# Rotary attention and MLP on one core: query-key scores as three pairs of 64-row products in place of four 128-row ones

## The reference, cut to what matters

```python
q_rot, k_rot = (rotate(q), rotate(k))
scores = scale * np.matmul(q_rot, k_rot.transpose(0, 1, 3, 2))
scores = scores - np.max(scores, axis=-1, keepdims=True)
attn = np.exp(scores)
attn = attn / (np.sum(attn, axis=-1, keepdims=True) + 1e-09)
x = attn @ v                       # heads side by side: 2304 x 512
h = x @ w_in                       # 512 x 2048
g = h * np.tanh(softplus(h))
out = g @ w_out                    # 2048 x 512
```

## Time and profile before

| what | value |
|---|---|
| median of 3 runs | 749.82 us (747.87 to 752.75) |
| profiled execution, its own time | 751.79 us |
| its span, first to last instruction | 750.0 us |
| mean granted TensorE clock | 0.993 of full |
| PE busy | 713.9 us, 95% |
| PE weight loads busy | 668.4 us, 89% |
| DVE busy | 482.9 us, 64% |
| ACT busy | 554.2 us, 74% |
| POOL busy | 350.0 us, 47% |
| scores, matmuls of line 577 | 640, busy 121.0 us in all |

### The profile page before, as it was taken

How to read it: one execution, slowest core, us unless ns; L and a number is a source line. 1 busy time by engine, 2 the same in 40 slices (tenths; PEclk the granted TensorE clock), 3 DMA queues, 4 the chain that set the end, 5 groups by cost and what they waited for, 6 DMA issues and landing times.

```text
span 750.0 us, 16092 instructions
## 1 busy us (share of the span) xinstructions
PE 713.9 (95%) x5098; PEld 668.4 (89%) x5098; DVE 482.9 (64%) x697; ACT 554.2 (74%) x999; POOL 350.0 (47%) x341
## 2 busy tenths in 40 slices
PE   1899999999999999889799999999999999999998
PEld 1799999999999999879699988999988999988996
DVE  4699999999999999977663433443443443533341
ACT  1799999999999999767777666656657567476653
POOL 4988888888888888761420303112031120301000
PEclk9999999999999999999899999999999999999999
DMA  3136633333333333365210202002020210200000
GB/s 86 41 75 189 189 81 80 79 78 79 77 74 80 80 81 80 82 193 192 84 29 29 85 29 57 28 30 81 28 84 0 84 28 28 84 28 0 0 28 28
DMA packets 89956, 52.30 MB, mean 70 GB/s; under 512 B 65456, under 2 KB 79408, under 8 KB 89936
## 3 DMA queue, kind: packets, MB, share of 16 engines
q1 hardware_dynamic: 89936, 52.03, 25.8%
HBM read 37.78 MB, written 14.23 MB: 69 GB/s over the span
## 4 chain that ended last, share of the span: by engine, by line
PE 85%; DVE 7%; issue 3%; ACT 3%; POOL 1%; DMA 0%; SPq 0%; DVEq 0%; POOLq 0%; ACTq 0%
PE ps_pv L614 11%; PE ps_s L577 9%; PE ps_t L595 9%; PE ps_y L698 9%; PE ps_y L699 9%; PE ps_y L700 9%; PE ps_h L680 8%; PE ps_h L679 8%; PE ps_h L678 8%; PE ps_t L563 4%; DVE neg_max L894 1%; DVE v_st L910 1%; DVE xt L920 1%; DVE gl L1003 1%; ACT prob L749 1%
## 5 line engine op out<-in xcount | busy, mean ns | idle before, releaser
L993 DVE TENSOR_TENSOR h_sb<-h_sb,m_sb 128x1024 f32<-128x1024 f32 x36 | 58.0, 1611 | 200.7 <-ACT m_sb L820 200.7
L680 PE MATMUL ps_h<-xb_h,win_lo 128*128 128x256 f32 x576 | 163.0, 283 | 0.0
L679 PE MATMUL ps_h<-xb_l,win_hi 128*128 128x256 f32 x576 | 163.0, 283 | 0.0
L678 PE MATMUL ps_h<-xb_h,win_hi 128*128 128x256 f32 x576 | 163.0, 283 | 0.0
L761 ACT ACTIVATE ph<-ps_t 128x320 fp32r<-128x320 f32 (+3 forms) x256 | 117.4, 470 | 12.5 <-PE ps_t L595 10.7
L595 PE MATMUL ps_t<-id_f,prob 128*128 128x128 f32 x800 | 125.3, 275 | 0.6 <-DVE rt_early L936 0.2
L894 DVE TENSOR_REDUCE neg_max<-ps_s 128x1 f32<-128x576 f32 (+1 forms) x160 | 119.1, 744 | 6.2 <-PE ps_s L577 6.2
L577 PE MATMUL ps_s<-qkt 128*128 128x288 f32 x640 | 121.0, 312 | 1.9 <-ACT prob L749 1.3
L749 ACT ACTIVATE prob<-ps_s,neg_max 128x576 f32<-128x576 f32 (+1 forms) x160 | 118.3, 739 | 3.8 <-DVE neg_max L894 2.9
L698 PE MATMUL ps_y<-wout_hi,gh 128*128 128x512 f32 x288 | 113.4, 394 | 4.2 <-DVE gl L1003 4.2
L614 PE MATMUL ps_pv<-ph,v_st 128*128 128x256 f32 (+1 forms) x320 | 106.8, 345 | 9.6 <-DVE xt L920 9.1
(11 more groups left out here) (63 smaller groups left out, 1306.7 us busy)
## 6 DMA issues: line engine op xcount, KB each, us to landing
x_transposed<-xt SPq DMA_DIRECT2D x64, 144.0 KB, 2.4
x_raw<-x_transposed SPq DMA_DIRECT2D x9, 512.0 KB, 4.0
x_more<-x_transposed SPq DMA_DIRECT2D x9, 512.0 KB, 4.9
x_more<-reciprocals SPq DMA_DIRECT2D x18, 256.0 KB, 3.7
v_raw<-v_in SPq DMA_DIRECT2D x32, 128.0 KB, 2.2
win_raw<-w_in SPq DMA_DIRECT2D x4, 1024.0 KB, 6.0
wout_raw<-w_out SPq DMA_DIRECT2D x4, 1024.0 KB, 9.1
y_out<-y_sb SPq DMA_DIRECT2D x8, 512.0 KB, 2.8
```

Of the source, the lines that this page charges most:

```text
L678: nc.tensor.matmul(o, wh, xb_h[:, c, :], start=(c == 0), stop=False)
L679: nc.tensor.matmul(o, wh, xb_l[:, c, :], start=False, stop=False)
L680: mm = nc.tensor.matmul(o, wl, xb_h[:, c, :], start=False, stop=(c == KC - 1))
```

## The change

The lo·lo product is left out. The three others are each made as a pair of products of 64 rows: the one on the upper 64 rows takes the first 288 keys, the one on the lower 64 rows the other 288. They write different PSUM banks. For this the queries lie as [hi; lo] and [lo; hi], the keys as [first half; second half], once high and once low. That gives six matmuls of 64 rows and 288 columns a query tile, each with its weight load, for four of 128 rows.

What else moves: `qk_st` becomes `q_st` and `k_st`; `Q` on POOL becomes five instructions in place of three (two copies, two subtractions, one copy, each of 320 values a partition, where two were of 640); `K3` has 6 transposes in place of 3; the copies out of PSUM write other places, with as many values; the columns that `T` reads are permuted; the first head's split on DVE has 5 instructions for 3, and one more small memset.

```diff
-        qk_st = sb1("qk_st", [P, 2, NT, 3, D], F32R)
+        q_st = sb1("q_st", [P, NT, 3, D], F32R)
+        k_st = sb1("k_st", [P, 2 * NT + 1, D], F32R)
...
-                nc.gpsimd.tensor_scalar(qk_st[:, :, :, 0, :], rot[:, e], 1.0, 1.0, ALU.mult,
-                                        ALU.mult).then_inc(qk_hi, 1)
-                pool.wait_ge(qk_hi, h)
-                nc.gpsimd.tensor_tensor(qk_st[:, :, :, 1, :], rot[:, e], qk_st[:, :, :, 0, :].bitcast(F32),
+                nc.gpsimd.tensor_scalar(q_st[:, :, 0, :], rot[:, e, 0], 1.0, 1.0, ALU.mult, ALU.mult).then_inc(qk_hi, 1)
+                nc.gpsimd.tensor_scalar(k_st[:, 0:NT, :], rot[:, e, 1], 1.0, 1.0, ALU.mult, ALU.mult).then_inc(qk_hi, 1)
+                pool.wait_ge(qk_hi, 2 * h - 1)
+                nc.gpsimd.tensor_tensor(q_st[:, :, 1, :], rot[:, e, 0], q_st[:, :, 0, :].bitcast(F32),
                                         ALU.subtract).then_inc(qk_parts, 1)
-                nc.gpsimd.tensor_scalar(qk_st[:, 0, :, 2, :], qk_st[:, 0, :, 0, :].bitcast(F32), 1.0, 1.0,
+                pool.wait_ge(qk_hi, 2 * h)
+                nc.gpsimd.tensor_tensor(k_st[:, NT:2 * NT, :], rot[:, e, 1], k_st[:, 0:NT, :].bitcast(F32),
+                                        ALU.subtract).then_inc(qk_parts, 1)
+                nc.gpsimd.tensor_scalar(q_st[:, :, 2, :], q_st[:, :, 0, :].bitcast(F32), 1.0, 1.0,
                                         ALU.mult, ALU.mult).then_inc(qk_parts, 1)
...
+                elif j == 2:
+                    for n, first in enumerate((0, 2, NT, NT + 2)):
+                        src = k_st[:, first:first + 2, :].rearrange("p t d -> p (t d)")
+                        mm = nc.tensor.transpose(bank[:, n * P:n * P + P], src, id_r[:])
+                else:
+                    for n, (low, part) in enumerate((low, part) for low in range(2) for part in range(3)):
+                        if part < 2:
+                            first = low * NT + 3 + part
+                            src = k_st[:, first:first + 2, :].rearrange("p t d -> p (t d)")
+                        else:
+                            src = q_st[:, 4, low:low + 2, :].rearrange("p a d -> p (a d)")
+                        mm = nc.tensor.transpose(bank[:, n * TAIL:n * TAIL + P], src, id_r[:])
...
-                for stack in range(2):
-                    for part in range(2):
-                        mm = nc.tensor.matmul(ps_s[:, buf, part, 0:S // 2], qkt[:, e, stack, t * P:t * P + P],
-                                              qkt[:, e, 2, part * (S // 2):(part + 1) * (S // 2)],
-                                              start=(stack == 0), stop=(stack == 1))
+                for n, (q_low, k_low) in enumerate(((0, 0), (0, 1), (1, 0))):
+                    for side in range(2):
+                        rows = slice(side * D, side * D + D)
+                        stack = q_low if side == 0 else 1 - q_low
+                        first = (D, HALF)[side]
+                        mm = nc.tensor.matmul(ps_s[:, buf, side, 0:S // 2],
+                                              qkt[rows, e, stack, Q_COL[t]:Q_COL[t] + P],
+                                              qkt[rows, e, k_low, first:first + S // 2],
+                                              start=(n == 0), stop=(n == 2))
...
-            nc.vector.tensor_copy(qk_st[:, :, :, 0, :], turned).then_inc(first_steps, 1)
+            nc.vector.tensor_copy(q_st[:, :, 0, :], turned[:, 0]).then_inc(first_steps, 1)
+            nc.vector.tensor_copy(k_st[:, 0:NT, :], turned[:, 1]).then_inc(first_steps, 1)
```

More of the change, by code:

```diff
@@ L54 @@
 NTB = 3
+K_FIRST = (0, 2 * P + TAIL, P, 3 * P + TAIL, 2 * P)
+QK_BLOCK = 320
+Q_COL = (384, 512, 704, 832, 640)
 def order(text):
@@ L231, in attention_mlp @@
         rot = sb1("rot", [P, 2, 2, NT, D])
-        qk_st = sb1("qk_st", [P, 2, NT, 3, D], F32R)
+        q_st = sb1("q_st", [P, NT, 3, D], F32R)
+        k_st = sb1("k_st", [P, 2 * NT + 1, D], F32R)
         v_raw = sb1("v_raw", [P, NT, D])
         v_st = sb1("v_st", [P, 2, NT, 2, D], F32R)
-        qkt = sb1("qkt", [P, 2, 3, NT * P], F32R)
+        qkt = sb1("qkt", [P, 2, 2, 3 * QK_BLOCK], F32R)
         id_f = sb1("id_f", [P, P])
@@ L444, in rotate @@
                 if due(h - 2):
-                    pool.wait_ge(qk_parts, 2 * (h - 2))
+                    pool.wait_ge(qk_parts, 3 * (h - 2))
                 nc.gpsimd.tensor_tensor(rot[:, e], part_c[:], part_s[:], ALU.add).then_inc(rope_done, 1)
@@ L556, in qk_turn @@
                     if due(h):
-                        pe.wait_ge(qk_parts, 2 * h)
+                        pe.wait_ge(qk_parts, 3 * h)
                     else:
[L559 to L563, removed]
+                        pe.wait_ge(first_steps, 9)
+                if j < 2:
+                    for t in range(4):
+                        src = q_st[:, t, j:j + 2, :].rearrange("p a d -> p (a d)")
+                        mm = nc.tensor.transpose(bank[:, t * P:t * P + P], src, id_r[:])
+                elif j == 2:
[10 more added lines that the diff above has]
+                        mm = nc.tensor.transpose(bank[:, n * TAIL:n * TAIL + P], src, id_r[:])
                 mm.then_inc(kt_done, 1)
@@ L592, in p_turn @@
                         col = j * nq + (qt - CHUNK_TILES[chunk][0]) * P
-                        first = min(kt * P, S - P)
+                        first = K_FIRST[kt] if kt < 4 else K_FIRST[4] - TAIL
                         src = prob[:, e, qt, first:first + P]
@@ L651, in _ @@
             pe.wait_ge(pads_cleared, 1)
-            pe.wait_ge(prob_pads, 1)
+            pe.wait_ge(prob_pads, 2)
             start, pairs, end = parts(PE_STEP)
@@ L733, in take_qk @@
                         act.wait_ge(s_done, NT * (h - 1))
+                blocks = qkt[:, e, :, :].rearrange("p a (b x) -> p a b x", x=QK_BLOCK)
                 src = ps_t[:, bank, :]
-                if j < 3:
-                    dst = qkt[:, e, j, 0:FULL]
-                else:
-                    src, dst = src[:, 0:3 * P].rearrange("p (a q) -> p a q", a=3), qkt[:, e, :, FULL:FULL + P]
+                if j == 0:
+                    src, dst = src.rearrange("p (b x) -> p b x", b=2), blocks[:, 0, 1:3, D:QK_BLOCK]
+                elif j == 2:
+                    src, dst = src.rearrange("p (a x) -> p a x", a=2), blocks[:, :, 0, D:QK_BLOCK]
+                else:
+                    src = src[:, 0:6 * TAIL].rearrange("p (a b x) -> p a b x", a=2, b=3)
+                    dst = blocks[:, :, :, 0:TAIL]
                 nc.scalar.activation(dst, src, ACT.Copy).then_inc(kt_taken_a, 1)
@@ L872, in _ @@
             dve.wait_ge(first_steps, 4)
-            nc.vector.tensor_copy(qk_st[:, :, :, 0, :], turned).then_inc(first_steps, 1)
-            dve.wait_ge(first_steps, 5)
-            nc.vector.tensor_tensor(qk_st[:, :, :, 1, :], turned, qk_st[:, :, :, 0, :].bitcast(F32),
+            nc.vector.tensor_copy(q_st[:, :, 0, :], turned[:, 0]).then_inc(first_steps, 1)
+            nc.vector.tensor_copy(k_st[:, 0:NT, :], turned[:, 1]).then_inc(first_steps, 1)
+            dve.wait_ge(first_steps, 6)
+            nc.vector.tensor_tensor(q_st[:, :, 1, :], turned[:, 0], q_st[:, :, 0, :].bitcast(F32),
                                     ALU.subtract).then_inc(first_steps, 1)
-            nc.vector.tensor_copy(qk_st[:, 0, :, 2, :], qk_st[:, 0, :, 0, :].bitcast(F32)).then_inc(first_steps, 1)
-            dve.wait_ge(first_steps, 7)
+            nc.vector.tensor_tensor(k_st[:, NT:2 * NT, :], turned[:, 1], k_st[:, 0:NT, :].bitcast(F32),
+                                    ALU.subtract).then_inc(first_steps, 1)
+            nc.vector.tensor_copy(q_st[:, :, 2, :], q_st[:, :, 0, :].bitcast(F32)).then_inc(first_steps, 1)
+            dve.wait_ge(first_steps, 9)
             nc.vector.memset(prob[TAIL:P, 1, 4, :], 0.0).then_inc(prob_pads, 1)
+            nc.vector.memset(k_st[:, 2 * NT, :].bitcast(F32), 0.0).then_inc(prob_pads, 1)
             dve.wait_ge(id_loaded, 16)
@@ L888, in take_q @@
                     dve.wait_ge(s_done, NT * (h - 1))
-                nc.vector.tensor_copy(qkt[:, e, 1, 0:FULL], ps_t[:, SLOT_OF["K", 1] % NTB, :]).then_inc(kt_taken_v, 1)
+                dst = qkt[:, e, 1, :].rearrange("p (b x) -> p b x", x=QK_BLOCK)[:, 1:3, D:QK_BLOCK]
+                nc.vector.tensor_copy(dst, ps_t[:, SLOT_OF["K", 1] % NTB, :].rearrange("p (b x) -> p b x", b=2)
+                                      ).then_inc(kt_taken_v, 1)
             def row_max(h, e, t):
```

## The result

The changed kernel takes 785.12 us (median of 4, 784.72 to 787.13) against 751.29 us before on the same chip: 1.0465 times as long, interval 1.0423 to 1.0508. The profiled execution has a span of 785.1 us against 750.0. The forecast was 744.0 with a range to 766: wrong in sign and outside the range.

The account below looks back on a forecast made before the run. PE, DVE and ACT were taken as near their limit together, POOL's loop bounding the new steps at 9.2 us. 751.8 - 7.5 (steps) + 0.5 (early steps) + 1.0 (start) = 745.8; against the median, 2 less, 744.0; range 738 to 766.

Parts of the forecast that it names:

- Three engines near the limit, so a saving is bounded: Attention stage: PE, DVE and ACT busy 98, 96 and 94 of 100 us; DVE's idle 4 bounds a saving.
- `v_lo` goes between two instructions of POOL and ends 0.35 behind the one that it met: DVE beside POOL: `v_lo` runs only between two POOL instructions, ending some 0.35 to 0.4 us after the one met.
- the two kinds of steps: Attention steps before: short ones of 9.0 us when `v_lo` meets POOL's first gap, long ones of 9.75 at the second.
- Scores: Score tiles on PE: pairs run together, 0.41 us a tile against 0.54, taking 0.5 from PE's part of the chain.
- rival A: Score tiles on PE: changing between 64 and 128 rows empties the array, 0.75 us a tile, 763 us; chance 0.25.
- the chain through DVE: Waits of a step: `xt` copy on DVE, PE from V3 to S1, M1 on DVE, `v_lo`; four score tiles on it.
- POOL's second gap: Gap after POOL's second `part_s`, 9.5 us after the last `v_lo`; a `v_lo` passing there makes a long step.
- Rival C: Score tiles on PE: the halves don't run together, 0.81 us a tile, +34 us, 783; chance 0.08.
- Transposes: K3 on PE: three more transposes, 0.22 us a step, hidden where PE waits 0.32 for `xt`.
- POOL's split: Split on POOL: 2.80 us becomes 3.0 to 3.1, +0.25; hidden after a long step, not after a short one.
- The start: First split on DVE, K3's slow start and PE's wait for the second head's split: +1.0 us in all, 0 to +1.5.

Follow-up runs that it names:

- before_three: The kernel before with three of a tile's four 128-row score products, on the old layout with POOL's and K3's old work: 744.4 us, ratio 0.9892.
- marked run: The changed kernel with its 64-row products ordered three upper, then three lower, the second and third lower cut to 256 columns: 784.2 us, a single run.

## Why the prediction was wrong, point by point

**Three engines near the limit, so a saving is bounded.** Right. A quarter of the score products left out, without any cost elsewhere, gives 1.1% (before_three), on 0.13 x 5 = 0.65 a step that PE saves in 9.48. The forecast's 0.8% was about all there was to win.

**`v_lo` goes between two instructions of POOL and ends 0.35 behind the one that it met.** Right as a mechanism: in the changed kernel `v_lo` ended 0.34 behind the `rot` that ended at 227.57, and 0.34 to 0.35 behind whatever it had to wait for in the other runs. The rule of the Trainium skill named in the prediction beside it ("SBUF — State Buffer", "SBUF: two separate sides") agrees. What was built on it wasn't borne out. With the tile at three pitches `v_lo` still took from 0.5 to 1.2 and the step 9.35, not 9.2. And the two kinds of steps, 9.0 and 9.75, are less sharp than the prediction has them: by the starts of `v_lo` the 27 steps before lie between 9.03 and 9.79, most of the short ones near 9.25.

**Scores.** This is the step that failed: "I take 0.41, since the halves share neither rows nor banks and nothing in the trace holds back matmuls that don't depend on each other". The streaming of it was right, three pitches. The price of changing between 64 and 128 rows was taken as nothing, and it is some 0.35 us for each way in and out: 0.36 by the run with one pair, 0.36 by the one with upper rows only, 0.75 for two (by the medians over the steps 0.34, 0.33 and 0.73). That is close to the upper bound of the prediction, 2 x 0.177. A tile is then 0.54 - 0.13 + 0.35 = 0.76, against the 0.75 of rival A.

The reason was wrong in kind: the trace of before couldn't show such a change, because it has not a single product of 64 rows; that it shows no hole between transposes and products of 128 rows says nothing on it. The rule of the Trainium skill that a change of tiling mode drains TensorE ("TensorEngine Tiling (Array Packing)", Key Properties) fits the price measured here, though no run shows the array empty, and with the price bounded by a row it deserved more than a quarter. The other rule of the Trainium skill, that products in different row groups start some 4 ns apart ("TensorE: Matmul & The Clock Gate", Part 3), was right too (3 to 10 ns by the records of the tile above). They don't contradict each other, and I had set them up as if one had to give way.

**Rival A** had the tile right and the time too low, 763. It counted the four tiles on the chain through DVE and let `v_lo` go through POOL's second gap. But PE's whole step grows by all five tiles and by the transposes. PE's own work in a step of before is 9.05 to 9.15 (from the run with two pairs); five times 0.22, and 0.25 for K3, make 10.40 to 10.50, and the run with the halved rotation, in which PE is never idle, has 10.45. A chain that is nearly level with another engine's whole step has to be priced on both. On top, `v_lo` came at 9.2 and 9.9 in turn, and at 9.9 stood behind `rot`: 10.66. The two parts: 777.5 - 751.3 = 26 us for PE, and the other 8 for `v_lo` behind `rot`.

**Rival C** gave 783 and has the time, with the wrong mechanism: the halves do run together. The time alone would have confirmed it; the starts of the records refute it.

**Transposes.** Six in 0.47 for three in 0.22: +0.25, near the 0.22. Hidden they weren't, as most of PE's wait for `xt`, their cover, had gone: between 100 and 300 us it adds up to 1.0 us, where it was 3.2.

**POOL's split.** 0.46, 0.46, 0.87, 0.87 and 0.46, from 227.84 to 230.81, 2.97 us for 2.80: the estimate was 3.0 to 3.1. It wasn't a bound: between 100 and 300 us `part_c` waited for its load in 12 of 19 steps.

**The start.** +1.0 was forecast. DVE's first split alone ended 1.6 later (15.00, where it had been 13.37). It began 0.4 later, and the last of its copies of 320 took 1.68 beside POOL's `rot`, where the first had taken 0.48:

```profile
13.32 1.68 DVE L910 CAST q_st<-q_st 128x320 fp32r<-128x320 f32 x1
...
16.16 1.23 PE L573 MATMUL ps_t<-id_r,q_st 128*128 128x128 f32 x8 [16.16 <-DVE id_r L915]
```

PE started at 16.16 where it had been 14.95, and by the second `v_lo` it was 5.2 late. The runs with four and three full products, which have all else of the change, were 2.2 and 3.3 late there, so some 2 to 3 are of the score tiles, and this isn't settled closer.

## What to carry to other kernels

On this chip two products of 64 rows in different halves do run in the time of one, but a stream that goes from 128-row work to 64-row work and back pays some 0.35 us each time, over two and a half matmuls of 288 columns. Three pairs in place of four full products save one pitch, 0.13, so by an estimate from these two numbers (0.35 / 0.13 tiles of three pairs) some eight pairs would have to stand together between two changes before the packing paid. No run tried that. Where the trace of before cannot show a thing at all, its silence is no evidence: take the bound from both sides, and see what the whole engine's step, not only the chain, does at the upper one.

## What the runs showed of the hardware

The two halves of the array's rows don't keep the program's order between them. The marked run started the program's fifth and sixth product ahead of its third. The Trainium skill says otherwise ("TensorE: Matmul & The Clock Gate", Part 3: matmuls keep the program's order in start and end); here the measurement decides, at least for products on different rows. One thing follows for code: in the marked run the product that carries the semaphore, the last in the program, began 0.007 us ahead of the third (218.506 and 218.513 by the records), so a signal on the last product alone need not mean that all are through (this is argued from the starts, and the last one was the shorter by 32 columns in that run; no run shows a reader that came too early).

The price of a change didn't depend on whether one half or both worked, nor on whether one pair or three stood between: 0.36 for one pair, 0.36 for upper rows alone, 0.35 for three pairs. It shows on the weight loads: the first one behind a change begins some 0.2 us later than in a stream of equal row counts.
